# A cross-engine relay at every tile, and four reorderings of queues, in a float32 attention and two-MLP kernel on one core

## The chip, the cores and the metric

The kernel runs on one core of one Trainium2 chip. The metric is the device time of one execution in microseconds (us), lower is better. The core has TensorE (PE, matrix products), VectorE (DVE), ScalarE (ACT), GpSimd (POOL) and SyncE (SP), which here issues all DMAs. Each engine works through its own queue in order; the queues meet only through semaphores.

## What is computed

Attention over channels, then two MLPs over 6016 tokens of width 256 with 2048 hidden units. The first MLP's gate is h·cos(h), the second's is h·sigmoid(h):

```python
qn = q / (norm(q, axis=1) + 1e-6); kn = k / (norm(k, axis=1) + 1e-6)
a = softmax(kn.T @ qn / tau)            # 256 x 256
x = v @ a
h = x @ w_in1;  x = (h * cos(h)) @ w_out1
h = x @ w_in2;  y = (h * sigmoid(h)) @ w_out2
```

All inputs and outputs are float32.

## The kernel before

**Products.** Every float32 product is made of three passes over operands split in a high and a low part (`three_passes`, L1235 to L1238: high·high, high·low, low·high). Each pass is one weight load of 128x128 and one matmul of 128 rows and n columns.

**Tiles and steps.** The tokens are cut in 12 tiles (`TILES`): the first has half-width n = 192, the other eleven n = 256. The hidden units are cut in 4 pieces (`STEPS`). A step q is one piece of one tile; steps 0 to 47 belong to the first MLP (`M1` = 48), steps 48 to 95 to the second. In tile t, step number s = q mod 4. The hidden layer of a step is computed as seven products in place of eight (`hidden(i, q)`, i = 1 to 7, six matmuls each), whose sums DVE and ACT assemble in a fixed chain. The output layer of the first MLP (`output1`) has eight groups of six matmuls a step, for the step three back; the output layer of the second (`output2`) has seven products of six, for the step two back. So a steady step is 90 matmuls in the first MLP and 84 in the second.

**The chain of a step.** After product 1, ACT copies it (`s1`, L476), and products 6 and 2 wait for that. After 6, ACT runs `s2` (L484), for which product 7 waits. After 7, ACT runs `s3` (L491), for which product 4 waits. DVE adds `c22` (L884) after 5 and `s3`, and product 3, at the start of the next step, waits for it; after 3, DVE adds `c12` (L891). In the first MLP ACT and DVE then make turns, phase, sine and gate and split the result; `lo_of_g` (L925) is the longest DVE instruction. In the second, ACT computes `silu` (L550) from `c12` and `c22`, and `silu_ps` (L561) from PSUM; then come the sums (`t13` L937, `t2`, `t4`) and splits (`hi_s` L573, `lo_s` L957, and so on).

**Once in a tile.** SP loads the input of tile t+2 (`load_form`, L319) once DVE has split that of tile t+1 (`lo_of_form`, L813), and stores the first MLP's result of tile t-1 (`store_x`, L323) once ACT has moved it out of PSUM (`move_x`, L538). In the step with s = 0 DVE needs the loaded input (`sums_of_form`, L790 to L802). ACT splits it (`hi_of_form`, L436). In the first MLP SP also loads, and stores in split form, the second MLP's weights.

**The relay.** At one place, L1329, PE waits for an instruction of POOL. In step q = 6 (`RELAYED`), PE ends product 1, starts `output1`, and, after the first three matmuls of its group 1, waits for `relay_done`. POOL waits for product 1 of that step and then writes a column of 128x1 zeros (L410), which nobody reads, and counts the semaphore up.

The order of everything is written out by hand: `first_mlp` and `second_mlp` of each engine give a step's order in the steady part, and lists of single calls stand for the beginning and for the passage from one MLP to the other.

Of the kernel before, what the change touches and what calls it, by code (L numbers as in the profile page):

```python
# [27 lines left out]
def channel_attention_two_mlps(nc: bass.Bass, qk, v_tiles, tau, w_in1, w_out1, w_forms2, y_tiles):  # L28
# [31 lines left out]
    def in1(q):  # L60
        return 0 <= q < M1
# [4 lines left out]
    def live(q):  # L66
        return 0 <= q < ALL


    RELAYED = STEPS + 2  # L70

    WP = 1024
    PIECES = KC * F // WP
# [9 lines left out]
    with ExitStack() as ctx:  # L83
# [69 lines left out]
        neg_max = sb("neg_max", [P, KC])  # L153
        row_sum = sb("row_sum", [P, KC])
        row_scale = sb("row_scale", [P, KC])
        relay = sb("relay", [P, 1])
        wr = [wr0, wr1, wr2, wr3]


# [127 lines left out]
        with nc.Block() as block:  # L287

            @block.sync
            def _(sp):  # L290
# [73 lines left out]
                for q in range(ALL + 4):  # L364
                    t, s = q // STEPS, q % STEPS
                    if s == 0:
                        if 3 <= t < 3 + 2 * STEPS:
                            store_w(t - 3)
                        if 2 <= t < 2 + 2 * STEPS:
                            load_raw(t - 2)  # L370
                    if q == 42:
                        sp.wait_ge(w_stored, 16 * 2 * STEPS)
                        load_w(0, 0)
                    if q == M1 - 2:
                        sp.wait_ge(p_done[3], M1 - 3)
                        load_w(0, 1)
                    if q == M1 - 1:
                        sp.wait_ge(p_done[3], M1 - 2)
                        load_w(0, 2)
                    if s == 3:  # L380
                        if t + 2 < 2 * TILES:
                            load_form(t + 2)
                        if 1 <= t <= TILES:
                            store_x(t - 1)
                        if TILES + 1 <= t:
                            store_y(t - TILES - 1)
                    if q == M1:
                        sp.wait_ge(p_done[3], M1 - 1)
                        load_w(1, 0)
                        sp.wait_ge(out_done[1], M1 - 3)  # L390
                        load_w(1, 1)
                    if q == M1 + 1:
                        sp.wait_ge(p_done[3], M1)
                        load_w(0, 3)
                        sp.wait_ge(out_done[1], M1 - 1)
                        load_w(1, 2)
                    if q == M1 + 2:
                        sp.wait_ge(out_done[1], M1)
                        load_w(1, 3)
                sp.wait_ge(y_stored, 16 * TILES)  # L400

            @block.gpsimd
            def _(pool):
                nc.gpsimd.memset(ident[:, :], 0.0).then_inc(ident_zeroed, 1)
                nc.gpsimd.memset(ones[:, :], 1.0).then_inc(consts_ready, 1)
                pool.wait_ge(ident_zeroed, 1)
                nc.gpsimd.affine_select(out=ident[:, :], in_=ident[:, :], compare_op=ALU.not_equal, fill=1.0,
                                        base=0, pattern=[[-1, P]], channel_multiplier=1).then_inc(consts_ready, 1)
                pool.wait_ge(p_done[1], RELAYED + 1)
                nc.gpsimd.memset(relay[:, :], 0.0).then_inc(relay_done, 1)  # L410

            @block.scalar
            def _(act):
# [239 lines left out]

                def second_mlp(q):
                    t, s = q // STEPS, q % STEPS
                    if s == 3 and TILES < t < 2 * TILES - 1:
                        hi_of_form(t + 1)
                    if in2(q - 1):
                        silu_ps(q - 1)
                    if in2(q - 2):  # L660
                        hi_24(q - 2)
                    if live(q):
                        s1(q)
                    if in2(q - 1):
                        silu(q - 1)
                    if s == 1 and t > TILES:
                        copy_out(t - TILES - 1)
                    if in2(q - 1):
# [564 lines left out]
            def _(pe):  # L1233
# [42 lines left out]
                def hidden(i, q):  # L1276
# [33 lines left out]
                                          i in (1, 5) and j == 0, True)  # L1310
                    mm.then_inc(p_done[i], 1)

                def output1(q, groups):
                    n, s, t, b = width(q), q % STEPS, q // STEPS, q % 2
                    for g in groups:
# [10 lines left out]
                        slot = 4 * b + {(0, 1): 0, (1, 1): 1, (1, 0): 2, (0, 0): 3}[odd, half]  # L1326
                        for j in range(2):
                            f = 2 * j + odd
                            if g == 1 and j == 1 and q + 3 == RELAYED:  # L1329
                                pe.wait_ge(relay_done, 1)  # L1330
                            cols = slice(d * P, (d + 1) * P)
                            mm = three_passes(banks[:, x_bank(t, d), half, 0:n], w1out[s][:, 0, f, cols],
                                              w1out[s][:, 1, f, cols], g_hi[:, slot, j, 0:n], g_lo[:, slot, j, 0:n],
# [5 lines left out]
                def output2(q, products):  # L1339
                    n, s, i = width(q), q % STEPS, q - M1  # L1340
                    t = i // STEPS
                    for o in products:
# [20 lines left out]
                                pe.wait_ge(y_step, 8 * (t - 1) + {2: 2, 5: 8, 6: 4}[o])  # L1363
                        at, half = OUT_AT[o]
                        for j in range(2):
                            mm = three_passes(banks[:, at, half, 0:n], o2w[s][:, 0, w - 1, j, :],
                                              o2w[s][:, 1, w - 1, j, :], g_hi[:, place, j, 0:n],
                                              g_lo[:, place, j, 0:n], s == 0 and o in FIRST_OF_BANK and j == 0,
                                              s == STEPS - 1 and j == 1)
# [33 lines left out]
                def first_mlp(q):  # L1403
# [12 lines left out]
                    hidden(2, q)  # L1416
                    hidden(5, q)
                    hidden(7, q)
                    output(3, 4, 5, 6)
                    hidden(4, q)  # L1420
                    output(7)

                def second_mlp(q):
                    def output(*products):
# [3 lines left out]
                    output(3)  # L1428
                    if live(q - 1):
                        hidden(3, q - 1)  # L1430
                    if live(q):
                        hidden(1, q)
                    output(1, 2, 7)
                    if live(q):
                        hidden(6, q)
                        hidden(5, q)
# [134 lines left out]
```

## Time and profile before

| | us |
|---|---|
| time, three runs | 1057.4, 1075.3, 1075.4; median 1075.3 |
| the profiled execution | 1075.3, of which the span is 1073.4 |
| PE matmul busy | 1052.2 (98%) |
| DVE busy | 954.6 (89%) |
| ACT busy | 807.9 (75%) |
| POOL busy | 0.9 |

The span runs from the first to the last instruction on the engines. PE is busy 98% of it, but its matmuls overlap: a matmul's shown duration (about 0.28 us) is its way through the array, and the next one starts about 0.11 to 0.12 us after it. What tells how fast PE goes is the distance between two starts, or the number of matmuls in a stretch, and not the busy share.

Columns: the view of stretches has the stretch, its length, and for each engine its busy time and, in brackets, the number of instructions, then the granted clock of TensorE (1.00 is 2.4 GHz), the DMA share and GB/s. The timeline has start, duration (us), engine, line, instruction, out<-in, shape, count, and in square brackets the engine's idle time before it and what ended it. The groups by shape have line, engine, instruction, names, shape, count, busy us, mean ns of one, and idle time before. A DMA row has out<-in, engine, count, KB each, and the median us from issue to landing.

### The profile page before, as it was taken

The numbers are of one execution on the slowest core, as the hardware profiler recorded it, in microseconds if no ns is written. First come the engines' busy times: TensorE is split into PE (matmuls) and PEld (weight loads), VectorE is DVE, ScalarE is ACT, GpSimd is POOL, SyncE is SP. The second block draws the span as 40 slices with busy tenths as digits, with TensorE's granted clock in tenths as the row PEclk, the third lists the DMA queues.
The fourth block names the chain that finished last, engine by engine and source line by source line (L and its number), as shares of the span: only waits on it lengthen the run. The fifth ranks groups of instructions, "written<-read, shape, count | busy, mean of one in ns | idle before, by whom it ended". The sixth has DMA issues, their size and how long they took to land. (4 is left out here: it accounts for less than half of the span.)

```text
span 1073.4 us, 21181 instructions
## 1 busy us (share of the span) xinstructions
PE 1052.2 (98%) x8718; PEld 1046.3 (97%) x8718; DVE 954.6 (89%) x1061; ACT 807.9 (75%) x875; POOL 0.9 (0%) x8
## 2 busy tenths in 40 slices
PE   7999999999999999999999999999999999999997
PEld 7979999999999999999999899999999999999997
DVE  7989989999999999998887489999999999999987
ACT  7778778778787778787777467877877777777775
POOL 0000000000000000000000000000000000000000
PEclk9999999999999999999999899999999999999999
DMA  8920011230230321203047211001101101101000
GB/s 282 308 61 21 21 35 55 77 126 21 108 128 21 109 96 53 109 26 153 35 158 281 86 37 36 34 8 40 41 2 41 40 2 41 40 2 40 21 21 20
DMA packets 18285, 76.03 MB, mean 71 GB/s; under 512 B 1808, under 2 KB 5904, under 8 KB 16144
## 3 DMA queue, kind: packets, MB, share of 16 engines
q1 hardware_dynamic: 18192, 74.72, 20.0%
q8 instruction: 67, 1.10, 0.4%
q14 instruction: 26, 0.21, 0.1%
HBM read 47.71 MB, written 27.00 MB: 70 GB/s over the span
## 5 line engine op out<-in xcount | busy, mean ns | idle before, releaser
L1238 PE MATMUL banks<-g_hi,w1out 128*128 128x256 f32 (+1 forms) x768 | 215.7, 281 | 0.0
L1236 PE MATMUL banks<-g_hi,w1out 128*128 128x256 f32 (+1 forms) x768 | 215.7, 281 | 0.0
L1237 PE MATMUL banks<-g_lo,w1out 128*128 128x256 f32 (+1 forms) x768 | 215.7, 281 | 0.0
L1236 PE MATMUL banks<-xf_hi,h1w 128*128 128x256 f32 (+1 forms) x672 | 190.1, 283 | 2.9 <-ACT banks L476 2.0
L1236 PE MATMUL banks<-g_hi,o2w 128*128 128x256 f32 (+1 forms) x672 | 188.8, 281 | 3.6 <-ACT xo L538 1.5
L1236 PE MATMUL banks<-xf_hi,h2w 128*128 128x256 f32 (+1 forms) x672 | 189.6, 282 | 1.9 <-ACT s_part L484 1.3
L1237 PE MATMUL banks<-xf_lo,h2w 128*128 128x256 f32 (+1 forms) x672 | 189.3, 282 | 0.0
L1238 PE MATMUL banks<-xf_hi,h2w 128*128 128x256 f32 (+1 forms) x672 | 189.3, 282 | 0.0
L1237 PE MATMUL banks<-xf_lo,h1w 128*128 128x256 f32 (+1 forms) x672 | 189.1, 281 | 0.0
L1238 PE MATMUL banks<-xf_hi,h1w 128*128 128x256 f32 (+1 forms) x672 | 189.1, 281 | 0.0
L1238 PE MATMUL banks<-g_hi,o2w 128*128 128x256 f32 (+1 forms) x672 | 188.6, 281 | 0.0
L1237 PE MATMUL banks<-g_lo,o2w 128*128 128x256 f32 (+1 forms) x672 | 188.6, 281 | 0.0
L1238 PEld LDWEIGHTS banks<-g_hi,w1out 128*128 128x128 f32 x768 | 147.7, 192 | 0.0
L1236 PEld LDWEIGHTS banks<-g_hi,w1out 128*128 128x128 f32 x768 | 144.9, 189 | 0.1
L1237 PEld LDWEIGHTS banks<-g_lo,w1out 128*128 128x128 f32 x768 | 145.0, 189 | 0.0
L1236 PEld LDWEIGHTS banks<-xf_hi,h1w 128*128 128x128 f32 x672 | 127.1, 189 | 4.2 <-ACT banks L476 2.6
L1236 PEld LDWEIGHTS banks<-g_hi,o2w 128*128 128x128 f32 x672 | 126.6, 188 | 4.4 <-issue 1.7
L1237 PEld LDWEIGHTS banks<-xf_lo,h2w 128*128 128x128 f32 x672 | 129.8, 193 | 0.0
L1238 PEld LDWEIGHTS banks<-xf_hi,h1w 128*128 128x128 f32 x672 | 129.6, 193 | 0.0
L1236 PEld LDWEIGHTS banks<-xf_hi,h2w 128*128 128x128 f32 x672 | 127.2, 189 | 2.2 <-ACT s_part L484 1.5
L1237 PEld LDWEIGHTS banks<-g_lo,o2w 128*128 128x128 f32 x672 | 129.1, 192 | 0.0
L1237 PEld LDWEIGHTS banks<-xf_lo,h1w 128*128 128x128 f32 x672 | 127.2, 189 | 0.1
(123 smaller groups left out, 2320.9 us busy)
## 6 DMA issues: line engine op xcount, KB each, us to landing
w_scr<-w_split SPq DMA_DIRECT2D x8, 1792.0 KB, 7.6
qk_raw<-qk SPq DMA_DIRECT2D x23, 512.0 KB, 4.7
h2w<-w_scr SPq DMA_DIRECT2D x4, 1792.0 KB, 7.9
o2w<-w_scr SPq DMA_DIRECT2D x4, 1792.0 KB, 8.2
form<-v_tiles SPq DMA_DIRECT2D x11, 512.0 KB, 3.6
x_scr<-xo SPq DMA_DIRECT2D x11, 512.0 KB, 2.6
form<-x_scr SPq DMA_DIRECT2D x11, 512.0 KB, 4.0
y_tiles<-xo SPq DMA_DIRECT2D x11, 512.0 KB, 4.9
```

Of the source, the lines that this page charges most:

```text
L1236: nc.tensor.matmul(out, w_hi, m_hi, start=start, stop=False, skip_group_check=True)
L1237: nc.tensor.matmul(out, w_hi, m_lo, start=False, stop=False, skip_group_check=True)
L1238: return nc.tensor.matmul(out, w_lo, m_hi, start=False, stop=stop, skip_group_check=True)
```

## The change

It does six things. (1) The relay, until now once, is made in 22 steps: the step s = 2 of every tile but the first, in both MLPs (`relayed`); POOL writes a column for each, and PE waits in the first MLP at the same place as before and in the second in the middle of output product 2. (2) In the steady first MLP PE does product 4 two output groups earlier. (3) In the steady second MLP PE does output product 1 ahead of hidden product 1 in place of behind it. (4) In the second MLP ACT does `silu` ahead of `s1`. (5) In the second MLP ACT does `hi_of_form` in step s = 2, not 3. (6) SP puts `store_x` ahead of `load_form`.

```diff
-    RELAYED = STEPS + 2
+    def relayed(q):
+        return q % STEPS == 2 and q // STEPS % TILES != 0
...
-        relay = sb("relay", [P, 1])
+        relay = sb("relay", [P, 2 * TILES])
... SP, in each step
                     if s == 3:
+                        if 1 <= t <= TILES:
+                            store_x(t - 1)
                         if t + 2 < 2 * TILES:
                             load_form(t + 2)
-                        if 1 <= t <= TILES:
-                            store_x(t - 1)
                         if TILES + 1 <= t:
                             store_y(t - TILES - 1)
... POOL
-                pool.wait_ge(p_done[1], RELAYED + 1)
-                nc.gpsimd.memset(relay[:, :], 0.0).then_inc(relay_done, 1)
+                for q in range(ALL):
+                    if relayed(q):
+                        t = q // STEPS
+                        pool.wait_ge(p_done[1], q + 1)
+                        nc.gpsimd.memset(relay[:, t:t + 1], 0.0).then_inc(relay_done, 1)
... ACT, second_mlp
-                    if s == 3 and TILES < t < 2 * TILES - 1:
+                    if s == 2 and t + 1 < 2 * TILES:
                         hi_of_form(t + 1)
                     if in2(q - 1):
                         silu_ps(q - 1)
                     if in2(q - 2):
                         hi_24(q - 2)
+                    if in2(q - 1):
+                        silu(q - 1)
                     if live(q):
                         s1(q)
-                    if in2(q - 1):
-                        silu(q - 1)
... PE
+                def wait_relay(q):
+                    t = q // STEPS
+                    pe.wait_ge(relay_done, t if t < TILES else t - 1)
... PE, output1
-                            if g == 1 and j == 1 and q + 3 == RELAYED:
-                                pe.wait_ge(relay_done, 1)
+                            if g == 1 and j == 1 and relayed(q + 3) and in1(q + 3):
+                                wait_relay(q + 3)
... PE, output2
                         for j in range(2):
+                            if o == 2 and j == 1 and relayed(q + 2) and live(q + 2):
+                                wait_relay(q + 2)
... PE, first_mlp
                     hidden(7, q)
-                    output(3, 4, 5, 6)
+                    output(3, 4)
                     hidden(4, q)
-                    output(7)
+                    output(5, 6, 7)
... PE, second_mlp
                         hidden(3, q - 1)
+                    output(1)
                     if live(q):
                         hidden(1, q)
-                    output(1, 2, 7)
+                    output(2, 7)
```

## Rows read from the trace of the kernel before

**Rows 1.** The page's busy times.

```profile
PE 1052.2 (98%) x8718; PEld 1046.3 (97%) x8718; DVE 954.6 (89%) x1061; ACT 807.9 (75%) x875; POOL 0.9 (0%) x8
```

**Rows 2.** Two long stretches, step 10 to 47 and step 54 to the end.

```profile
167.00:568.30 401.30, 401.30 (x3410) 401.30 (x3409) 364.16 (x338) 310.46 (x303) 0.00 (x0) 1.00 0.24 86
642.50:1060.80 418.30, 418.30 (x3554) 418.30 (x3553) 385.37 (x462) 322.47 (x359) 0.00 (x0) 1.00 0.08 26
```

**Rows 3.** Timeline of PE at the end of the second MLP, around a wait.

```profile
1060.53 0.28 PE L1236 MATMUL banks<-g_hi,o2w 128*128 128x256 f32 x1
...
1061.47 0.28 PE L1238 MATMUL banks<-g_hi,o2w 128*128 128x256 f32 x1
1062.74 0.39 PE L1236 MATMUL banks<-g_hi,o2w 128*128 128x256 f32 x1 [1.00 <-DVE g_lo L957]
1062.97 0.28 PE L1237 MATMUL banks<-g_lo,o2w 128*128 128x256 f32 x1
...
1064.80 0.28 PE L1238 MATMUL banks<-g_hi,o2w 128*128 128x256 f32 x1
```

**Rows 4.** Timeline of PE, between the MLPs, first and last of 29.

```profile
594.52 0.28 PE L1237 MATMUL banks<-g_lo,w1out 128*128 128x256 f32 x1
...
597.69 0.28 PE L1238 MATMUL banks<-g_hi,w1out 128*128 128x256 f32 x1
```

**Rows 5.** Timeline of PE and POOL at the one relay.

```profile
124.62 0.28 PE L1238 MATMUL banks<-xf_hi,h1w 128*128 128x256 f32 x1
...
124.96 0.10 POOL L410 MEMSET relay<- 128x1 f32 x1 [123.49 <-PE banks L1238]
...
125.11 0.36 PE L1236 MATMUL banks<-g_hi,w1out 128*128 128x192 f32 x1
...
125.31 0.27 PE L1237 MATMUL banks<-g_lo,w1out 128*128 128x192 f32 x1
```

**Rows 6.** Groups by shape: 127 to 128.9 us, then 132 to 132.3.

```profile
L1238 PE MATMUL banks<-xf_hi,h1w 128*128 128x256 f32 x7 | 1.9, 276 | 0.0
...
L1238 PE MATMUL banks<-xf_hi,h1w 128*128 128x256 f32 x2 | 0.6, 281 | 0.0
```

**Rows 7.** Timeline of DVE, ACT and weight loads, one step, first MLP.

```profile
303.54 0.69 DVE L891 TENSOR_TENSOR h<-banks,s_part 128x512 f32<-128x512 f32 x1 [0.61 <-PE banks L1238]
...
314.14 0.69 DVE L891 TENSOR_TENSOR h<-banks,s_part 128x512 f32<-128x512 f32 x1 [0.61 <-PE banks L1238]
...
309.38 0.59 ACT L491 ACTIVATE s_part<-banks 128x512 f32<-128x512 f32 x1
...
311.71 0.19 PEld L1236 LDWEIGHTS banks<-xf_hi,h1w 128*128 128x128 f32 x1
```

**Rows 8.** Timeline of DVE, then ACT, then weight loads, second MLP.

```profile
810.21 0.69 DVE L891 TENSOR_TENSOR h<-banks,s_part 128x512 f32<-128x512 f32 x1 [0.34 <-PE banks L1238]
...
810.92 0.58 ACT L476 ACTIVATE banks<-banks 128x512 f32<-128x512 f32 x1
811.41 1.05 ACT L550 ACTIVATE work<-h 128x1024 f32<-128x1024 f32 x1
...
812.73 0.19 PEld L1236 LDWEIGHTS banks<-xf_hi,h2w 128*128 128x128 f32 x1
```

**Rows 9.** DMA issues, then SP's store and DVE's need of the load.

```profile
form<-v_tiles SPq DMA_DIRECT2D x11, 512.0 KB, 3.6
...
y_tiles<-xo SPq DMA_DIRECT2D x11, 512.0 KB, 4.9
...
312.28 0.33 SPq L323 DMA_DIRECT2D x_scr<-xo  x1
...
317.01 0.69 DVE L790 TENSOR_TENSOR form<-form 128x512 f32<-128x512 f32 x1
```

**Rows 10.** Stretches around the passage between the MLPs.

```profile
585.00:590.00 5.00, 3.11 (x27) 2.77 (x25) 3.30 (x4) 3.62 (x4) 0.00 (x0) 1.00 0.75 264
590.00:595.00 5.00, 5.00 (x30) 5.00 (x31) 1.02 (x2) 0.81 (x1) 0.00 (x0) 0.66 0.24 103
```

## Prediction, made before the changed kernel was run

> **What bounds the kernel now.** I read the page's busy times first: PE is at 98%, DVE at 89%, ACT at 75% [rows 1]. The list of waits by total time leaves PE almost nothing between 107 and 585 us, and nothing between 610 and 1061 us. So PE's own stream sets the time, and a change helps only if it makes PE issue faster or takes one of the few stalls away. The busy share cannot say how fast PE issues. The view of stretches can: 3410 matmuls in 401.3 us and 3554 in 418.3 us [rows 2], 117.7 ns from start to start in both. A steady step of 90 matmuls therefore takes 10.60 us, one of 84 takes 9.89 us; DVE's rows of one step in the first MLP, 303.54 and 314.14, stand just that far apart [rows 7].
>
> Next the timeline of PE, where a stall interrupts it. Before the wait at 1061.47 us eight distances take 0.94 us: 117.5 ns each. After it (1.00 us idle, first distance 0.23 us) sixteen distances take 1.83 us, 114.4 ns each with the settling in it [rows 3]. These are the same instructions on the same shapes at the same granted clock. At 594.52 to 597.69 us, also behind stalls, 28 distances take 3.17 us, 113.2 ns [rows 4]. The groups by shape show the two as well, in the mean duration: 276 ns against 281 ns. There, 256-wide products run at 276 shortly after the relay and at 281 again at 132 us, once some products of the 192-wide tile lie between [rows 6]. So for 256 columns PE has two regular paces, 113.3 and 117.8 ns. It was in the slower all through both long stretches, which held no stall that could have changed it. A stall is followed by the faster one in each of these three places. The runs fit with that: one of the three is 17.9 us shorter, and one MLP at the faster pace would be worth about 16 us (below).
>
> **The relays.** (a) Their price. At the one relay PE ended the third matmul of the group and should have started the next 4 x 0.113 = 0.45 us after 124.62; it started at 125.11, 0.49 after, and the following one 0.20 us later in place of 0.11 [rows 5]: 0.04 + 0.09 = 0.13 us, and with the settling of [rows 3] (0.23 in place of 0.113 us, and some 0.01 more) 0.17 us. I take 0.15. There are 11 relayed steps in each MLP and one is there already: 21 x 0.15 = 3.2 us (2.7 to 3.6). POOL has nothing else to do, and each writes 0.10 us. Behind the waiting weight load stand all of PE's later products; `s1`, which ACT runs in this time, only gains slack.
> (b) Their yield. If each relay leaves PE at the faster pace and it holds to the next (four steps, all of 256 columns), the stretch from the relay of step 10 (167 us) to 568.3 us shrinks by 4.5/117.8, taken as 3.77%: 15.1 us. The stretch from step 54 (642.5 us) to 1060.8 us shrinks by 15.8 us. Sum 30.9 us. What lies before 167 us and between 568 and 642 us mixes 192 with 256 columns; I count nothing there (at best 1.8 us more, at 133 to 167 us and in the last of the passage).
> The Trainium skill ("TensorE: Matmul & The Clock Gate", section "Wait — 56ns, not 53.3ns?") has one warm distance only, N / 2.4 GHz plus about 2.5 ns, whatever came before: 109.2 ns at 256 columns, by its figures. The trace disagrees twice, with 113.2 and 117.7 ns [rows 2, 4]. By that rule a pause has no yield, and the change would cost what its relays cost; that is rival 1 below.
>
> **Can the others keep up?** First MLP: in the fullest steps DVE's only idle time in 10.60 us is 0.61 us [rows 7]. The faster step takes 90 x 4.44 ns = 0.40 us of it, so 0.21 us stay. Second MLP: the tightest step leaves DVE 0.34 us of 9.89 [rows 8], the faster pace wants 84 x 4.44 ns = 0.37 us, so DVE falls behind by 0.03 us in that step and catches up in the others: over the whole stretch it is idle 32.9 of 418.3 us, 0.78 us a step on average [rows 2]. Both MLPs are just feasible. The price of the 0.03 us, were it not covered, is 11 x 0.03 = 0.3 us; I count 0.
>
> **The reorderings.** Product 4 two groups (12 matmuls, 1.41 us) earlier: `s3` ends at 309.97, the weight load of product 4 was at 311.71 and comes at 310.30 [rows 7]. The slack falls from 1.74 to 0.33 us, and at the faster pace to some 0.2 us: no stall. It lets ACT read products 2 and 4 sooner, which helps only an ACT or DVE that is late: 0.
> Output product 1 ahead of hidden product 1, and `silu` ahead of `s1`: `c12` is ready at 810.21 + 0.69 = 810.90 and `silu` takes 1.05 us, so `s1` starts at 811.95, not 810.92, and ends at 812.53. Product 6 loads at 812.73, which is unchanged, because as many matmuls stand ahead of it as before [rows 8]. Slack 0.2 us, and 0.1 us at the faster pace. The sums of the second MLP can start earlier on DVE. Gain 0; loss 0 to 0.1 us in each of 46 steps if it does not fit. I take 0, since it fits by the rows.
> `hi_of_form` a step earlier moves 1.69 us of ACT from one step to the one before, of the same shape: 0. Its input was summed two steps ahead.
> `store_x` ahead of `load_form`: in the step with s = 3 the load now leaves SP only when ACT has moved the result, 312.28 + 0.33 = 312.6 us, half a step later than before. Alone it lands 3.6 us after its issue, at 316.2; behind another transfer, as `y_tiles` is now, 4.9 us, at 317.5. DVE asks for it at 317.01 [rows 9]. So DVE waits 0 to 0.5 us (0 to 0.8 at the faster pace) in ten tiles. DVE's idle time there, 0.61 us in the step before it [rows 7], takes most of it. I count 0.1 us each, 1 us in all (0 to 5). The 1.8 MB of split weights and the next raw weights go behind it and have a whole tile's time.
> The passage between the MLPs (585 to 610 us) keeps its hand-written lists and its waits: 0, with 2 us either way.
>
> **Sum.** Against the profiled execution, 1075.3 us, which is also the median: 1075.3 - 30.9 + 3.2 + 1.0 = 1048.6 us. The span is 1.9 us less. The likeliest case's own range: gain 30.9 to 32.7, relays 2.7 to 3.6, the load 0 to 5, passage ±2, so 1043 to 1055.
>
> **The rivals.**
> 1. The relays do not do it: the pace after a relay is 117.8 ns again within a few products. For: at 132 us it was lost after the one relay there is, and this relay was never tried in a stretch of 256 columns alone. Against: there the 192-wide products came between; in [rows 3, 4] nothing falls back. Time: 1075.3 + 3.2 + 1.0 = 1079.5 us.
> 2. One MLP only: DVE or ACT at their limits of 0.03 to 0.2 us stall PE as often as the pace gains, most likely in the second MLP, where `s1` now waits for `silu`. Then 1075.3 - 15.1 + 3.2 + 1.0 = 1064.4 us.
> 3. The other side: the granted clock falls at relays. In the passage PE idles about 1.9 us at 585 to 590 us, and then the clock is 0.66 over 5 us with 30 matmuls in place of 44 [rows 10]: about 1.6 us lost each time. For: a relay is a pause too. Against: the one relay's pause was some 0.1 us and the clock stayed at 1.00. Should every one of 21 do it, with the pace not improved: 1079.5 + 34 = 1113 us. It decides from about 11 relays on (17 us more, 1096.8, is 2% over).
>
> **How the numbers follow.** Chances: likeliest case 0.60, a better one than its range 0.03, one MLP or a part 0.20, no effect 0.13, the clock or another loss beyond 2% 0.04. The range goes from 1043 to 1067 us: it holds the likeliest case and the second rival, and leaves out 0.03 + 0.13 + 0.04. About 2% is what a measurement of this kernel can tell from no change, 1053.8 us on the faster side. Most of the likeliest case lies below that, but it is a near thing, since one of the runs of before took 1057.4 us: I give faster 0.55, within 2% 0.41, slower 0.04.
>
> **What the changed profile would show.** Right: mean durations of 276 ns for the 256-wide matmuls in both MLPs, some 3540 in the first stretch's 401.3 us; 22 rows of the POOL line, each followed by a distance of about 0.20 to 0.23 us on PE; PE still at 98%. Wrong: 281 ns behind a relay (rival 1); stalls on `s1`, on `s3` or on the form's landing in every tile (rival 2); a granted clock under 1.00 outside the passage (rival 3).

## The result, and the profile after

The changed kernel took 1064.8 us in the median of 20 runs (1057.2 to 1068.6); the kernel before took 1072.8 us in the median of its 20 (1056.3 to 1075.5). The median fell by 8.0 us, 0.7%; 1048.6 us was predicted, 2.5% less. Nine runs of before lie at 1056 to 1060 us and eleven at 1073 to 1076, nothing between, and a ratio is taken against the nine shorter ones alone: it is 1.006, with an interval of 1.004 to 1.007, no change by the 2% bound, and a little slower. Of the changed kernel's runs 19 lie in the middle, at 1061 to 1069 us, and one at 1057. What this means is a part of what had to be found out.

The page's span and first row of busy times of the changed kernel (profiled execution 1067.4 us, 7.9 less than before's):

```profile
span 1065.5 us, 21202 instructions
...
PE 1043.8 (98%) x8718; PEld 1035.7 (97%) x8718; DVE 954.7 (90%) x1061; ACT 805.2 (76%) x875; POOL 3.0 (0%) x29
```

PE is at 98% as in [rows 1]; nothing here says where the expected 26 us are. The groups by shape do. Behind 130 us the 256-wide matmuls have a mean of 276 ns at the faster pace and 281 ns at the slower [rows 6]; before, 75 of 7541 were fast. After, 2205 of 3846 are fast in the first MLP and 1244 of 3695 in the second, 3449 in all. So the relays do something, but for under half of the matmuls, and fewest in the second MLP.

The view of stretches shows in which pieces, against one unbroken slow stretch in each MLP in [rows 2]. Each row below lies within one piece between two changes. A matmul lasts 0.28 us and is counted in every stretch that it touches, so about two are to be taken off: 234 in 26.5 us are 113 ns from start to start, 95 in 11.2 us are 118 ns.

```profile
168.70:195.20 26.50, 26.50 (x236) 26.50 (x235) 24.97 (x22) 22.03 (x23) 0.00 (x0) 1.00 0.32 118
197.20:208.40 11.20, 11.20 (x97) 11.20 (x97) 10.24 (x12) 8.69 (x9) 0.00 (x0) 1.00 0.00 0
210.40:236.90 26.50, 26.50 (x236) 26.50 (x236) 25.14 (x22) 22.20 (x22) 0.00 (x0) 1.00 0.33 121
251.40:291.90 40.50, 40.50 (x346) 40.50 (x346) 37.29 (x35) 32.12 (x32) 0.00 (x0) 1.00 0.23 86
720.00:755.00 35.00, 35.00 (x299) 35.00 (x298) 32.46 (x36) 26.05 (x31) 0.00 (x0) 1.00 0.10 31
...
855.70:873.00 17.30, 17.30 (x149) 17.30 (x149) 15.37 (x17) 14.02 (x17) 0.00 (x0) 1.00 0.01 1
```

Three kinds of boundary stand between such pieces. The timeline shows each.

*A relay that leaves PE slow.* The relays at 209.85 and at 250.86 us, with POOL's column at the first of them; columns as in [rows 3].

```profile
209.84 0.10 POOL L414 MEMSET relay<- 128x1 f32 x1 [41.53 <-PE banks L1242]
...
209.85 0.28 PE L1242 MATMUL banks<-g_hi,w1out 128*128 128x256 f32 x1
209.99 0.39 PE L1240 MATMUL banks<-g_hi,w1out 128*128 128x256 f32 x1
210.22 0.28 PE L1241 MATMUL banks<-g_lo,w1out 128*128 128x256 f32 x1
...
250.86 0.28 PE L1242 MATMUL banks<-g_hi,w1out 128*128 128x256 f32 x1
251.01 0.39 PE L1240 MATMUL banks<-g_hi,w1out 128*128 128x256 f32 x1
251.23 0.28 PE L1241 MATMUL banks<-g_lo,w1out 128*128 128x256 f32 x1
```

The first came out of a slow piece and left PE fast; the second came out of a fast piece and left it slow. To the eye the two are alike: 0.14 and 0.15 us to the waiting matmul, 0.23 and 0.22 us to the next. (The rows are rounded to 10 ns. By the trace's unrounded starts the second distance is 222 ns at the first relay and 226 ns at the second.)

*A pause on `c22`.* DVE waited 0.85 us for the tile's input, was late with `c22` (L888), and product 3 came 0.09 us late. The fast piece ends here, and the 11.2 us piece at 118 ns follows.

```profile
191.19 0.69 DVE L794 TENSOR_TENSOR form<-form 128x512 f32<-128x512 f32 x1 [0.85 <-DMA form<-v_tiles]
...
196.05 0.68 DVE L888 TENSOR_TENSOR h<-banks,s_part 128x512 f32<-128x512 f32 x1
...
196.59 0.28 PE L1242 MATMUL banks<-g_hi,w1out 128*128 128x256 f32 x1
196.79 0.39 PE L1240 MATMUL banks<-xf_hi,h1w 128*128 128x256 f32 x1
197.02 0.28 PE L1241 MATMUL banks<-xf_lo,h1w 128*128 128x256 f32 x1
```

*No pause at all.* In the second MLP the pace falls in five places (659.6, 698.6, 777.2, 855.9 and 934.5 us), each two steps behind a relay, where no distance is above 0.125 us. There `silu_ps` (L565) has waited for DVE, `silu` (L554) is now next, and `s1` (L480) ends at 659.47; the weight load of product 6 (L1240), which waits for it, starts at 659.52, 0.12 us behind the load ahead of it and about 8 ns late.

```profile
656.06 1.03 ACT L565 ACTIVATE work<-banks 128x1024 f32<-128x1024 f32 x1 [1.76 <-DVE work L955]
657.93 1.05 ACT L554 ACTIVATE work<-h 128x1024 f32<-128x1024 f32 x1
658.88 0.59 ACT L480 ACTIVATE banks<-banks 128x512 f32<-128x512 f32 x1
...
659.40 0.19 PEld L1242 LDWEIGHTS banks<-g_hi,o2w 128*128 128x128 f32 x1
659.52 0.19 PEld L1240 LDWEIGHTS banks<-xf_hi,h2w 128*128 128x128 f32 x1
```

The list of waits (who waits, for what: us in all, how often, the longest) and the row of the load answer to [rows 9]:

```profile
DVE form L794 <- DMA form<-v_tiles: 6.1, 9, 0.9
...
DVE form L794 <- DMA form<-x_scr: 1.9, 1, 1.9
```

```profile
form<-v_tiles SPq DMA_DIRECT2D x11, 512.0 KB, 4.9
```

**The account.** Product 1 of a step marks the same work in both traces.

| between product 1 of steps | before, us | after, us | difference |
|---|---|---|---|
| start to 6 | 124.6 | 125.6 | +1.0 |
| 6 to 47 (first MLP) | 434.4 | 427.1 | -7.3 |
| 47 to 54 (passage) | 83.4 | 86.2 | +2.8 |
| 54 to 95 (second MLP) | 405.6 | 402.0 | -3.6 |
| 95 to the end | 25.4 | 24.6 | -0.8 |

By causes: 3374 more fast matmuls at 4.44 ns each are -15.0 us; the pauses between matmuls cost 3.9 us more; the start, the passage and the rest are +3.2. The sum is -7.9. Against the forecast, half of the pace's 30.9 us is missing.

### The profile page after: what moved, and what is told of

It is laid out like the page before. It is cut to its first block and busy times, and to the rows that moved or that the text cites. A ratio compares the mean times of both kernels' runs of the same rounds, so it can differ in the third digit from the quotient of the medians.

```text
span 1065.5 us, 21202 instructions
## 1 busy us (share of the span) xinstructions
PE 1043.8 (98%) x8718; PEld 1035.7 (97%) x8718; DVE 954.7 (90%) x1061; ACT 805.2 (76%) x875; POOL 3.0 (0%) x29
## 5 line engine op out<-in xcount | busy, mean ns | idle before, releaser
L1240 PE MATMUL banks<-g_hi,w1out 128*128 128x256 f32 (+1 forms) x768 | 214.5, 279 | 0.0
L1241 PE MATMUL banks<-g_lo,w1out 128*128 128x256 f32 (+1 forms) x768 | 213.4, 278 | 0.0
L1240 PE MATMUL banks<-g_hi,o2w 128*128 128x256 f32 (+1 forms) x672 | 189.6, 282 | 3.6 <-DVE g_lo L967 1.6
L1240 PE MATMUL banks<-xf_hi,h1w 128*128 128x256 f32 (+1 forms) x672 | 189.6, 282 | 2.9 <-ACT banks L480 1.9
L1240 PE MATMUL banks<-xf_hi,h2w 128*128 128x256 f32 (+1 forms) x672 | 189.1, 281 | 2.6 <-ACT s_part L488 1.3
L1240 PEld LDWEIGHTS banks<-g_hi,w1out 128*128 128x128 f32 x768 | 144.4, 188 | 0.7
L1240 PEld LDWEIGHTS banks<-g_hi,o2w 128*128 128x128 f32 x672 | 128.1, 191 | 5.2 <-DVE g_lo L967 2.1
L1240 PEld LDWEIGHTS banks<-xf_hi,h1w 128*128 128x128 f32 x672 | 127.9, 190 | 4.7 <-ACT banks L480 2.6
L1240 PEld LDWEIGHTS banks<-xf_hi,h2w 128*128 128x128 f32 x672 | 128.5, 191 | 3.2 <-ACT s_part L488 1.5
L1242 PEld LDWEIGHTS banks<-xf_hi,h1w 128*128 128x128 f32 x672 | 128.9, 192 | 0.0
```

The costliest lines, as they stand in the source:

```text
L1240: nc.tensor.matmul(out, w_hi, m_hi, start=start, stop=False, skip_group_check=True)
L1241: nc.tensor.matmul(out, w_hi, m_lo, start=False, stop=False, skip_group_check=True)
L1242: return nc.tensor.matmul(out, w_lo, m_hi, start=False, stop=stop, skip_group_check=True)
```

## The experiments

Each kernel is told as a change to the kernel before or to the changed kernel. The three groups (first four, next four, last three kernels) ran beside their own runs of before, whose medians were 1059.1 (15 runs), 1072.8 (7) and 1071.7 us (11): how many runs of before fall near 1057 differs that much. The ratios of the second group stand against runs of before at 1072 to 1075 us, those of the other two against runs at 1055 to 1060 us, so ratios of different groups are not to be compared, and the traces carry the argument more than the medians do. One execution of each kernel was profiled.

**The relays alone.** The changed kernel with all reorderings undone; 22 relays in before's orders.

```diff
+    def relayed(q):
+        return q % STEPS == 2 and q // STEPS % TILES != 0
...
-                            if g == 1 and j == 1 and q + 3 == RELAYED:
+                            if g == 1 and j == 1 and relayed(q + 3) and in1(q + 3):
...
+                            if o == 2 and j == 1 and relayed(q + 2) and live(q + 2):
+                                wait_relay(q + 2)
```

> All five reorderings undone, the 22 relays kept. Theory K (a pause at the slower pace puts PE on the faster, a pause at the faster mostly puts it back, and the small waits for the form's load and for s1 put it back too): no waits of DVE for form, no pause on c22 in the step behind it; fast and slow stretches change only at relays, so about half the 256-wide matmuls of each MLP run at 276 ns, time 1060 to 1066 us. Rival R (each pause draws the pace at random, whatever went before): the same share, but with relays out of a fast stretch that stay fast as often as not. Rival S (the reorderings cost time by themselves): 1055 us or less.

Ten runs: five at 1046.3 to 1053.0 us, five at 1065.8 to 1068.6; median 1059.4, ratio 0.997 (0.992 to 1.003). The stretches of the profiled one (span 1044.4 us):

```profile
166.60:205.40 38.80, 38.80 (x344) 38.80 (x344) 37.00 (x36) 31.83 (x31) 0.00 (x0) 1.00 0.25 89
412.30:452.60 40.30, 40.30 (x344) 40.30 (x343) 37.16 (x35) 32.03 (x31) 0.00 (x0) 1.00 0.24 86
627.00:1030.00 403.00, 403.00 (x3558) 403.00 (x3558) 385.82 (x463) 321.09 (x359) 1.08 (x11) 1.00 0.09 27
```

In the first MLP a fast piece now lasts until a relay ends it: between relays nothing falls. Six relays in a row leave PE fast, the seventh (411.6 us) leaves it slow for a whole tile. In the second MLP the relays make no pause at all. In before's order product 1 stands ahead of output product 1, so nine matmuls lie between the end of product 1 and the waiting one, and POOL's column is ready long before; POOL writes its 11 columns in the row. The faster pace, entered in the passage, held there for 403 us: 3556 matmuls at 113.3 ns. That the second lump of runs, 18 us above, is the same kernel with the slower pace drawn at that one place fits in size with the 15.8 us of the prediction, but no such run was profiled.

**The reorderings alone.** The changed kernel with the one relay of before, in step 6.

```diff
+    RELAYED = (6,)
     def relayed(q):
-        return q % STEPS == 2 and q // STEPS % TILES != 0
+        return q in RELAYED
```

> The five reorderings kept, the relay only in step 6 as before. Theory K: nothing but the waits for form can change the pace in the first MLP and nothing in the second, so mostly 281 ns, time as before, 1070 to 1077 us, or about 16 us less in executions that happen to enter one MLP at the faster pace. Rival S: slower than before by 3 us or more beyond that.

Four runs, 1074.0 to 1077.0 us, ratio 1.019 (1.016 to 1.021). The slower pace in both MLPs:

```profile
132.50:566.00 433.50, 433.50 (x3683) 433.50 (x3682) 392.21 (x367) 332.27 (x326) 0.00 (x0) 1.00 0.22 81
639.00:1058.00 419.00, 419.00 (x3560) 419.00 (x3560) 385.95 (x463) 320.29 (x359) 0.00 (x0) 1.00 0.08 26
```

None of the four came out near 1057, where nine of the fifteen runs of before beside it did. The reorderings thus cost some 2 us against the longer times of before beside them (1072 to 1075 us), and they take away its shorter ones, as far as four runs can tell. How they do that is argued and not shown here, since this kernel was never at the faster pace. The reason offered is what the changed kernel and the next ones show: with `silu` ahead of `s1` a weight load comes late in most tiles of the second MLP in which PE is fast, and the faster pace ends there.

**Relays in steps 6, 10 and 54 only, in before's orders.** PE waits at the changed kernel's places.

```diff
-    RELAYED = STEPS + 2
+    RELAYED = (6, 10, 54)
...
```

> The kernel before with relays in steps 6, 10 and 54 only: one in each MLP's stretch of 256 columns, nothing that knocks PE out again. Theory K: both relays come at the slower pace and give the faster, which then holds for the whole stretch: 276 ns in both MLPs, about 3400 and 3550 matmuls, 1075.3 - 30.9 + 0.3 = 1045 us. Rival R: each MLP is fast in some executions and slow in others: 1045, 1060 or 1075 us. Rival S2 (at the faster pace DVE or ACT can't keep up and knock PE back within a few tiles even without the reorderings): 1055 to 1070 us with pauses on c22 or s1.

Four runs: 1042.9, 1058.9, 1059.9 and 1061.6 us. The profiled one (1059.9):

```profile
169.00:553.60 384.60, 384.60 (x3395) 384.60 (x3395) 362.13 (x337) 309.31 (x302) 0.00 (x0) 1.00 0.25 89
625.00:1044.00 419.00, 419.00 (x3560) 419.00 (x3560) 385.75 (x464) 322.85 (x360) 0.10 (x1) 1.00 0.08 26
```

The relay of step 10 gives the first MLP its faster pace for 3393 matmuls without a break, where eleven relays gave 2205 in the changed kernel. In the second MLP the relay made no pause, as above, and PE stayed slow. The run at 1042.9 would be the one in which the passage left PE fast.

**The load ahead of the store.** The changed kernel with SP's order of before.

```diff
                     if s == 3:
-                        if 1 <= t <= TILES:
-                            store_x(t - 1)
                         if t + 2 < 2 * TILES:
                             load_form(t + 2)
+                        if 1 <= t <= TILES:
+                            store_x(t - 1)
```

> The changed kernel with load_form ahead of store_x again. Theory K: DVE's nine waits for the form (6.1 us in all) go, and so do the pauses on c22 that ended the fast stretch in five tiles of the first MLP; but the next relay then comes at the faster pace and mostly ends it itself, so the share of 276 ns in the first MLP stays between 45 and 65% and the time within 3 us of the changed kernel's. Rival F (the form's wait is what the change lost in the first MLP): fast share over 90% there, 6 to 7 us less.

Median of six 1066.1 us, ratio 1.009 (1.006 to 1.012): not faster than the changed kernel. DVE's wait for the input is gone and with it all pauses on `c22`, which in the changed kernel had ended the faster pace at 197, 322 and 364 us (three tiles, and not five as I had written). Yet:

```profile
167.50:206.30 38.80, 38.80 (x345) 38.80 (x344) 37.15 (x35) 31.71 (x31) 0.00 (x0) 1.00 0.25 89
208.40:248.80 40.40, 40.40 (x345) 40.40 (x345) 37.29 (x35) 32.01 (x31) 0.00 (x0) 1.00 0.24 85
```

In the first MLP whole tiles alternate, fast and slow, and the relays do it: 1810 fast to 2035 slow. So the late load is not what holds the changed kernel back. The second MLP, where nothing of this edit applies, again falls without a pause two steps behind relays, here six times.

**`s1` ahead of `silu`.** The changed kernel with ACT's order of before there.

```diff
-                    if in2(q - 1):
-                        silu(q - 1)
                     if live(q):
                         s1(q)
+                    if in2(q - 1):
+                        silu(q - 1)
```

> The changed kernel with s1 ahead of silu again, all else kept (relays in the second MLP still pause). Theory K (silu ahead of s1 makes product 6 wait some 8 ns for s1, two steps behind a relay, and that alone puts PE back on 117.8 ns): the falls to 281 ns without any pause go, and the second MLP changes its pace at relays only; its share of 276 ns rises from 34% to 50% or more. Rival R (the pace falls back by itself after some 165 matmuls): the share stays near 34%.

1052.6, 1057.5, 1057.5 and 1061.5 us, ratio 0.985 (0.982 to 0.988). In the second MLP the falls without a pause are gone; 2987 of 3695 matmuls of the second MLP are fast, where it was 1244. One fast stretch of it, and then a pause that is new:

```profile
636.20:666.30 30.10, 30.10 (x268) 30.10 (x267) 28.27 (x31) 22.75 (x27) 0.00 (x0) 1.00 0.11 32
```

```profile
667.78 0.28 PE L1242 MATMUL banks<-g_hi,o2w 128*128 128x256 f32 x1
667.97 0.39 PE L1240 MATMUL banks<-xf_hi,h2w 128*128 128x256 f32 x1
```

In the step in which ACT also copies the output (`copy_out`), product 7 now waits for `s2`, 0.18 to 0.19 us in place of 0.11. Eight such pauses met a fast PE, and all eight left it fast; in the two tiles where PE came slow the load was only some 20 ns late, and PE was fast behind it. So it is not the length of a wait that costs here: this kernel's pauses take 5.6 us from step 10 to 47 and 54 to 95, the changed one's 3.9, and it is 7 us faster in the median.

**One pause in each MLP.** Before, with output product 1 ahead of hidden product 1 in the second MLP (which gives the relay its pause) and relays in steps 10 and 54.

```diff
-    RELAYED = STEPS + 2
+    RELAYED = (10, 54)
...
+                    output(1)
                     if live(q):
                         hidden(1, q)
-                    output(1, 2, 7)
+                    output(2, 7)
```

> The kernel before, with output product 1 ahead of hidden product 1 in the second MLP (so that a relay there is a real pause) and relays in steps 10 and 54 only. Theory K: the first MLP is at 276 ns from step 10 to 47 in every execution. The second enters step 54 at either pace, as in the kernel before: from the slower the pause gives the faster (1043 us), from the faster it mostly gives the slower (1059 us). Rival R: the outcomes of before, 1057 and 1075 us, occur too.

1048.0, 1059.4, 1063.8 and 1067.3 us, ratio 0.982 (0.976 to 0.988).

```profile
168.60:553.40 384.80, 384.80 (x3398) 384.80 (x3397) 362.30 (x337) 309.31 (x302) 0.00 (x0) 1.00 0.25 89
631.80:664.80 33.00, 33.00 (x283) 33.00 (x282) 30.07 (x35) 26.21 (x30) 0.00 (x0) 1.00 0.10 29
```

The first MLP is fast throughout again. PE came into the relay of step 54 fast and left it slow; later, distances of 130 ns, again behind a slightly late load for product 7, lifted the pace three times (665, 901 and 979 us) and pauses of about 0.06 us on product 7 ended it three times (703, 939 and 1017 us), 1050 fast to 2645 slow. A relay that meets a fast PE is a risk, and so is output product 1 ahead of hidden product 1.

**Relays in 6, 10 and 54 in the changed kernel.**

```diff
+    RELAYED = (6, 10, 54)
     def relayed(q):
-        return q % STEPS == 2 and q // STEPS % TILES != 0
+        return q in RELAYED
```

> The changed kernel with all its reorderings and relays in steps 6, 10 and 54 only. Theory K: each MLP is put on the faster pace once and put back within two to three steps, the first by the pause on c22 behind the form's late load, the second by s1; both then stay at 281 ns: 1072 to 1076 us. Rival R: as the run with three relays without the reorderings, 1043 to 1060 us.

1065.1 to 1074.5 us, ratio 0.997 (0.993 to 1.000).

```profile
167.60:439.00 271.40, 271.40 (x2394) 271.25 (x2393) 259.20 (x244) 219.98 (x214) 0.00 (x0) 1.00 0.24 88
441.00:557.00 116.00, 116.00 (x987) 116.00 (x986) 100.83 (x92) 87.70 (x88) 0.00 (x0) 1.00 0.23 81
634.00:1049.00 415.00, 415.00 (x3526) 415.00 (x3525) 382.22 (x455) 316.33 (x355) 0.00 (x0) 1.00 0.08 26
```

I had expected the pauses on `c22` to end the faster pace within a few steps; it outlived three of them (at 236, 318 and 359 us) and fell for good at the one at 441 us. With 22 relays such a fall lasts to the next relay, with three it lasts to the end. In the second MLP the relay left PE slow, and it stayed so.

**Longer pauses.** The orders of the kernel with one pause each, 22 relays, and PE waits three matmuls earlier.

```diff
-                            if g == 1 and j == 1 and q + 3 == RELAYED:
+                            if g == 1 and j == 0 and relayed(q + 3) and in1(q + 3):
...
+                            if o == 2 and j == 0 and relayed(q + 2) and live(q + 2):
```

> As e8, but with all 22 relays and the wait three matmuls earlier, so that each pause is about 0.34 us longer (7.5 us in all). Theory K with the outcome set by where in a clock cycle PE starts again: another length gives another rule, for instance faster after every pause (1050 us) or slower after every pause (1082 us), and the first distance after the pause tells which. Theory K without it: strict alternation as in the changed kernel, 1067 us.

1058.5 to 1069.9 us, ratio 0.993 (0.989 to 0.998). A stretch of each MLP behind such a relay, and PE's waits:

```profile
166.00:204.60 38.60, 38.60 (x343) 38.60 (x342) 36.84 (x35) 31.27 (x31) 0.00 (x0) 1.00 0.25 89
...
673.50:704.30 30.80, 30.80 (x274) 30.80 (x273) 28.97 (x33) 24.56 (x29) 0.00 (x0) 1.00 0.10 36
```

```profile
PE banks L1240 <- POOL relay L414: 5.7, 22, 0.3
```

The waiting matmul now comes 0.49 us behind the one ahead of it in the first MLP and 0.58 us in the second. Of 20 such pauses met at the faster pace 19 kept it (8 of 9 in the first MLP, 11 of 11 in the second), where the short ones kept it in 16 of 34. 3310 of 3846 and 3551 of 3695 matmuls are fast, nearly the forecast's share; but the pauses take 12.6 us from step 10 to 47 and 54 to 95, against 3.9 in the changed kernel, so the time is no better. The pace needs few pauses, not many.

**Two longer pauses.** Before, no relay in step 6, relays in 10 and 54, PE waiting directly behind product 1 in both MLPs. No reordering at all.

```diff
-    RELAYED = STEPS + 2
+    RELAYED = (10, 54)
...
-                            if g == 1 and j == 1 and q + 3 == RELAYED:
+                            if g == 1 and j == 0 and relayed(q + 3) and in1(q + 3):
...
+                            if o == 1 and j == 0 and relayed(q + 2) and live(q + 2):
+                                wait_relay(q + 2)
```

> The kernel before with two relays only, in steps 10 and 54, each wait directly behind product 1 (the longer pause, about 0.4 us, also in the second MLP), none in step 6. Theory L (a pause of this length gives 113.3 ns whatever the pace before, and without the reorderings nothing ends it): both MLPs at 276 ns nearly always, median 1043 us, ratio to before about 0.975 to 0.985. Theory K (a pause at the faster pace puts it back): half the executions 1043, half 1059 us.

1042.9, 1043.2, 1044.2, 1044.2, 1045.1 and 1057.1 us: median 1044.2, the best of all kernels here and 2.6% under the median of before beside it (1071.7); ratio 0.990 (0.984 to 0.995), which stands against before's shorter runs. Its page gives a span of 1042.3 us and PE busy 1020.4 of them, 98% again. Its stretches:

```profile
167.00:552.00 385.00, 385.00 (x3399) 385.00 (x3399) 362.20 (x337) 309.23 (x302) 0.00 (x0) 1.00 0.25 89
627.50:1028.80 401.30, 401.30 (x3543) 401.30 (x3542) 384.00 (x458) 319.30 (x357) 0.00 (x0) 1.00 0.09 27
```

7056 of 7541 matmuls are fast. Two pauses, and no late load from step 10 to 47 and 54 to 95: against the profiled execution of before the time is 31.1 us less (1075.3 to 1044.2), the size of the pace's gain that the prediction summed, 30.9 us, and here without the cost of 22 relays. The waits of PE for POOL that the list shows are 0.5 us together. Both pauses met a slow PE in this execution, so it does not test whether a longer pause keeps the faster pace.

**Two short pauses.** The same with the wait three matmuls later (`j == 1` in both).

> As the run before it with the short pause (three matmuls between product 1 and the wait). Theory K: the first MLP fast always if it arrives at step 10 at the slower pace, the second fast or slow by the pace at which it arrives at step 54: 1043 or 1059 us. Theory L makes no difference to the first MLP.

1044.4, 1045.3, 1057.1 and 1059.6 us, ratio 0.995 (0.987 to 1.003). The profiled one is fast in both (3417 of 3846, 3582 of 3695):

```profile
628.00:1028.80 400.80, 400.80 (x3539) 400.80 (x3538) 383.81 (x459) 319.22 (x357) 0.00 (x0) 1.00 0.09 27
```

Two of its four runs are some 14 us longer, against one of six with the longer pauses. That speaks for the longer pause and does not prove it.

**Two longer pauses and the store first.** The kernel with two longer pauses, and on SP the changed kernel's order.

```diff
                     if s == 3:
-                        if t + 2 < 2 * TILES:
-                            load_form(t + 2)
                         if 1 <= t <= TILES:
                             store_x(t - 1)
+                        if t + 2 < 2 * TILES:
+                            load_form(t + 2)
```

> The two long pauses again, with store_x ahead of load_form, the change's order on SP. Theory W (DVE's wait for the form's load makes PE pause on c22, and some of these pauses end the faster pace for good, as none comes to restore it): nine waits for the form, first MLP partly at 281 ns, 3 to 15 us more than the same without it; the second MLP as there. Rival: the wait is hidden, same time.

1051.2, 1057.4, 1059.6 and 1072.4 us, ratio 0.999 (0.994 to 1.004), 14 us above its twin in the median. In the profiled one:

```profile
167.00:193.00 26.00, 26.00 (x232) 26.00 (x231) 24.17 (x22) 21.34 (x22) 0.00 (x0) 1.00 0.32 116
195.50:566.00 370.50, 370.50 (x3148) 370.50 (x3147) 336.00 (x314) 285.84 (x279) 0.00 (x0) 1.00 0.23 82
640.50:1042.00 401.50, 401.50 (x3545) 401.50 (x3544) 384.19 (x459) 319.36 (x357) 0.00 (x0) 1.00 0.09 27
```

```profile
DVE form L796 <- DMA form<-v_tiles: 5.5, 9, 0.8
```

The first tile's late input made `c22` late (it ended at 194.87 us) and product 3 with it: it started at 194.92, 167 ns behind the matmul ahead of it, about 0.05 us late, and that ended the faster pace of the whole first MLP: 259 of 3846 fast. The second, without a store of this kind, is whole. This is the cleanest price of all: between the two profiled executions a lateness of 0.05 us on PE cost 13 us. It need not have ended the pace: of 18 pauses on `c22` that met a fast PE in four profiled kernels (this one, the changed one, `s1` ahead of `silu`, and three relays in the changed kernel), 0.01 to 0.24 us late, 10 ended it and 8 did not, and the longest of them did not.

## Why the prediction went wrong, step by step

**What held.** *Two paces.* 113.3 and 117.8 ns are real, last for thousands of matmuls, and either can run in either MLP: 3556 matmuls in 403 us in one kernel, 3558 in 419 us in another. DVE and ACT follow at the faster one; in the kernel with two longer pauses PE waits for neither from step 10 to 47 and 54 to 95. *The relay's price.* 0.15 us was taken; five start-to-start distances (0.142, 0.222, 0.120, 0.116 and 0.116 us, 0.716 in all, where five at the faster pace take 0.566) put it at 0.15. The sum by which the prediction came to it read the one relay of before a little wrong: one of the four distances behind 124.62 us follows a 192-wide matmul and is 0.09 us, so that pause was 0.07 us and not 0.04. *The clock.* It stayed at 1.00 at every relay of both MLPs; the third rival fell. *The first rival* fell too: it was to bring 281 ns again within a few products, and one relay gave 3393 fast matmuls. With it falls what it rested on, the Trainium skill's single warm distance for back-to-back matmuls ("TensorE: Matmul & The Clock Gate", section "Wait — 56ns, not 53.3ns?"): an estimate by its figures gives 109.2 ns at 256 columns. The traces, with a weight load ahead of each matmul, show 113.3 and 117.8 ns and neither is that one.

**The step that failed: "each relay leaves PE at the faster pace and it holds to the next".** Both halves did. I had three places where a stall was followed by the faster pace [rows 3, 4, 6] and took that as what a stall does. One of them [rows 3] shows PE coming from the slower pace. Another [rows 6] is no evidence of a yield at all, because the trace of before has PE at the faster pace ahead of the one relay, whose waiting matmul starts at 125.11 us. Its timeline shows four distances in 0.45 us, 112.5 ns each:

```profile
122.90 0.28 PE L1238 MATMUL banks<-xf_hi,h1w 128*128 128x256 f32 x1
...
123.35 0.25 PE L1236 MATMUL banks<-g_hi,w1out 128*128 128x192 f32 x1
```

At 120.16 to 120.64 us four such distances take 0.48 us. Between the two there is no relay, only the change between products of 192 and 256 columns. Over the 80 short pauses at relays in 256-wide stretches of all the profiled kernels, 39 of 46 that met a slow PE left it fast, but only 16 of 34 that met a fast PE left it so. A relay is good for a slow PE and harmful for a fast one. With 22 of them the pace is drawn anew in each tile; I costed a repetition as if it could only confirm.

**"I take 0, since it fits by the rows."** For `silu` ahead of `s1` the prediction found 0.1 us of slack at the faster pace, and bounded a miss at 0.1 us a step. The slack is used up where `silu_ps` waits for DVE first, a wait that this sum, worked out from one step of [rows 8], did not have in it. The miss was 8 ns. What was wrong is the price: not 8 ns but the pace of all that follows. The five slow pieces behind them last 18.6, 58.3, 58.3, 58.3 and 58.4 us, to the next relay or, where that one left PE slow, to the one after it: 251.9 us, 2140 matmuls at 4.44 ns, 9.5 us. With `s1` put back, 1743 more matmuls of the second MLP were fast: 7.7 us.

**"I count 0.1 us each, 1 us in all (0 to 5)" for the load behind the store.** DVE's wait measured 6.1 us in nine tiles, 0.7 us each, inside the 0 to 0.8 us that the prediction gave for the faster pace, and the transfer took 4.9 us, as the row of `y_tiles` let expect. Again the wait on DVE is not the price. It reached PE as 0.01 to 0.15 us on product 3. In the changed kernel that cost little that the relays did not already cost (its removal brought nothing); alone, beside a held pace, it cost 13 us.

**The passage, "0, with 2 us either way".** It is 2.8 us longer, and so outside. Two things make this up. PE's distances above 0.3 us there sum to 7.0 us in place of 5.8: DVE waits 1.9 us for an input read back from `x_scr`, whose load the store now delays, and PE waits 0.68 us for `c22`; PE's wait for `g_lo` grows from 1.0 to 1.6 us, and that for `xo` shrinks. The wait for `c22` is gone with SP's order put back; that for `g_lo` is 1.6 us in each kernel that has output product 1 ahead of hidden product 1, also in those with no other reordering, and 1.0 us in each without.

```profile
572.57 0.35 PE L1240 MATMUL banks<-xf_hi,h2w 128*128 128x192 f32 x1 [0.68 <-DVE h L888]
```

The rest is the clock. Behind these waits the granted clock is below 1.00 for a while, as in [rows 10]. Stretches of the changed kernel:

```profile
590.00:600.00 10.00, 8.37 (x57) 8.12 (x56) 3.25 (x4) 3.87 (x6) 0.00 (x0) 0.80 0.50 184
600.00:610.00 10.00, 9.07 (x59) 8.94 (x58) 4.54 (x7) 4.50 (x8) 0.00 (x0) 0.69 0.14 54
```

The part of the clock that is missing, times the length, is 2.0 and 3.1 us here; before it was 1.7 and 1.5 us in the same two and 0.2 in the next, where it is 0 now: 5.1 against 3.4 us, 1.7 us more. The start, 1.0 us longer, has the same: 0.84 in place of 0.91 from 60 to 80 us. Two other kernels (three relays, and one pause in each MLP) show 0.84 there as well and all the rest 0.91, so part of this is chance and not the change. The third rival looked for a falling clock at the relays and found none; where PE already idled, it fell for longer.

**The baseline.** The prediction set before against its slow median and read the 17.9 us between its three runs as what one MLP at the faster pace is worth. It did not follow it up: if before draws a pace by chance, then a change is measured against a mixture, and may lose the good draws. The runs fit with that. Nine of 20 runs of before lie near 1057 us, and none of the reorderings' four; 19 of the changed kernel's 20 lie above 1061. That is why the median falls by 0.7% while against before's shorter runs the time is 0.6% longer. That before's runs near 1057 us have the second MLP fast, and not the first, is inferred from kernels that differ from it only by relays; none of them was profiled.

**The second rival** gave nearly the right time, 1064.4 us for 1064.8, and named `s1` behind `silu` in the second MLP. Its mechanism, stalls that take as much time as the pace gains, is not what happened: the stalls took 3.9 us, and the pace was lost, in both MLPs. That the time lies inside the stated range, 1043 to 1067 us, and 0.4 us from this rival's, is luck.

## What to carry to other kernels

When PE is at 98%, look at start-to-start distances and at how many matmuls stand in equal stretches; a gain or a loss of 4% can hide there. A pace that depends on history is a state: ask of each repeated wait what it does to an engine in the good state, not only in the bad one, and make one deliberate pause where a long regular stretch begins rather than one in every tile. In such a stretch price a lateness by what it ends and not by its length, and leave some slack ahead of every wait of PE.

## What the runs showed of the hardware

The next pace can be read from the second distance at a short relay's pause, the one behind the waiting matmul, in unrounded starts: at 224 ns or less PE was fast behind it in 55 of 55, at 225 or more slow in 25 of 25. Behind a pause on `c22` this does not hold: in the kernel with the store first the distance was 221 ns, and PE was slow. A relay in which the waiting matmul came 0.49 or 0.58 us behind the one ahead of it kept the faster pace in 19 of 20 (the kernel with 22 longer pauses), one of 0.15 us in 16 of 34.

A weight load that comes some 8 to 11 ns late at the faster pace (a matmul distance of 122 to 124 ns) ended the faster pace without any pause, in five places of the changed kernel and in six of the one with the load first. One that comes about 20 ns late at the slower pace (loads 137 to 139 ns apart, the next matmul distance 130 or 131 ns) did the opposite in the kernel with `s1` first, at 707.6 and 747.1 us, and at three places of the kernel with one pause in each MLP, and lifted the slower pace to the faster; in four other tiles of the latter, with loads 134 to 136 ns apart and a distance of 124 or 125 ns, PE stayed slow. Why distances this close together should lead to different paces is open, and no run here tests a reason. Open too is what the earlier `hi_of_form` and the earlier product 4 do by themselves; they were not tried alone. In the first MLP the relays alone and the load first differ only by product 4's place: the relays that met a fast PE kept the pace in 5 of 7 there and in 0 of 5 here, one profiled execution each, which points at product 4's place and proves nothing.
